# Maxima, squares and x in another order around the late joins of a fused attention and MoE kernel

## The reference

```python
for t in range(S):                       # attention: S = 768, 4 batches, 8 heads, D = 48
    S_re, S_im = (ar * S_re - ai * S_im + kv), (ar * S_im + ai * S_re)   # a normed to |a| <= 0.999
    y[:, :, t] = einsum('bhd,bhde->bhe', q[:, :, t], S_re)
x = y as (3072 tokens, 384)
h = maximum(maximum(x @ w1, x @ w2), x @ w3)    # 384 -> 768
x2 = h @ w_out                                  # 768 -> 384
expert = argmax(softmax(norm(x2) @ norm(emb).T / tau))   # 8 experts
out = gate * (relu(x2 @ e1[expert]) @ e2[expert])        # 384 -> 1024 -> 384
```

## Time and profile before

| | |
|---|---|
| median of three runs | 951.6 us |
| profiled execution | 952.29 us |
| its span | 950.6 us |
| mean granted TensorE clock | 0.948 |
| TensorE matmul busy | 841.3 us, 89% |
| VectorE busy | 662.6 us, 70% |
| GpSimd busy | 509.0 us, 54% |
| ScalarE busy | 441.8 us, 46% |

### The profile page before, as it was taken

How to read it: one execution, slowest core, us unless ns; L and a number is a source line. 1 busy time by engine, 2 the same in 40 slices (tenths; PEclk the granted TensorE clock), 3 DMA queues, 4 the chain that set the end, 5 groups by cost and what they waited for, 6 DMA issues and landing times.

```text
span 950.6 us, 18638 instructions
## 1 busy us (share of the span) xinstructions
PE 841.3 (89%) x6641; PEld 775.1 (82%) x6642; DVE 662.6 (70%) x1066; ACT 441.8 (46%) x817; POOL 509.0 (54%) x886
## 2 busy tenths in 40 slices
PE   0548898879898999999999999976999999999995
PEld 0436787779787988988888998875999999998894
DVE  5968898789888999999978756337623353647831
ACT  5676755646555556666543434221412132436611
POOL 1294989699997989899986000001332232324222
PEclk9777999989999999999999999995999999999998
DMA  9401141352424243423221111134721015245411
GB/s 305 110 20 31 29 141 64 91 142 73 111 72 105 74 106 100 107 69 92 77 60 39 40 41 48 48 115 157 280 69 50 33 52 183 66 152 204 144 34 42
DMA packets 41874, 89.72 MB, mean 94 GB/s; under 512 B 6264, under 2 KB 23680, under 8 KB 40480
## 3 DMA queue, kind: packets, MB, share of 16 engines
q1 hardware_dynamic: 37632, 76.04, 26.3%
q0 software_dynamic: 4160, 12.60, 4.0%
HBM read 69.74 MB, written 17.69 MB: 92 GB/s over the span
## 4 chain that ended last, share of the span: by engine, by line
PE 59%; DVE 22%; ACT 7%; issue 7%; DMA 2%; SPq 2%; ACTq 0%; DVEq 0%; POOL 0%; POOLq 0%
PE mm L1686 7%; PE mm L1690 6%; PE mm L1687 6%; PE yu L1686 4%; PE yu L1690 4%; PE yu L1687 4%; PE sc L1743 2%; DVE l_im L1136 2%; DVE l_re L1135 2%; PE tr L1954 2%; DVE h_sb L1155 2%; PE tr L1955 2%; PE mm L1955 2%; PE yu L1784 2%; PE mm L1954 2%
## 5 line engine op out<-in xcount | busy, mean ns | idle before, releaser
L1686 PE MATMUL mm<-up_hi,x_hi 128*128 128x384 f32 x432 | 159.3, 369 | 26.7 <-DVE h_sb L1155 13.7
L1687 PE MATMUL mm<-up_lo,x_hi 128*128 128x384 f32 x432 | 149.9, 347 | 0.0
L2053 POOL TENSOR_TENSOR c_re<-ring 112x128 f32<-112x128 f32 x165 | 101.3, 614 | 81.8 <-DVE ring L1108 48.3
L2054 POOL TENSOR_TENSOR c_im<-ring 112x128 f32<-112x128 f32 x165 | 119.0, 721 | 0.0
L1686 PEld LDWEIGHTS mm<-up_hi,x_hi 128*128 128x128 f32 x432 | 83.3, 193 | 41.7 <-DVE h_sb L1155 16.1
L2133 POOL DMA_INDIRECT out_rows<-g_o,rows_out x30 | 36.0, 1200 | 146.5 <-DVE g_o L1538 139.0
L1690 PE MATMUL mm<-up_hi,x_lo 128*128 128x384 f32 x432 | 102.3, 346 | 0.0
L2057 POOL TENSOR_TENSOR ring<-c_re,c_im 112x64 f32<-112x64 f32 x165 | 96.8, 586 | 0.0
L2109 POOL DMA_INDIRECT g_in<-x_scratch,rows_in x34 | 38.4, 1130 | 103.1 <-DVE rows_in L1501 77.6
L2056 POOL TENSOR_TENSOR ring<-c_re,c_im 112x64 f32<-112x64 f32 x165 | 80.5, 488 | 12.9
L1155 DVE TENSOR_TENSOR h_sb<-mm,h_sb 128x384 f32<-128x384 f32 x96 | 52.9, 552 | 49.2 <-PE mm L1690 47.1
(11 more groups left out here) (263 smaller groups left out, 2254.8 us busy)
## 6 DMA issues: line engine op xcount, KB each, us to landing
raw<-in_moe_w SPq DMA_DIRECT2D x16, 1536.0 KB, 9.2
a_dn<-in_a_laid SPq DMA_DIRECT2D x18, 384.0 KB, 6.9
an_scratch<-a_dn SPq DMA_DIRECT2D x18, 384.0 KB, 2.3
ring<-an_scratch SPq DMA_DIRECT2D x18, 384.0 KB, 5.3
q_in<-in_q_laid SPq DMA_DIRECT2D x24, 224.0 KB, 3.0
k_in<-in_k_laid SPq DMA_DIRECT2D x24, 224.0 KB, 3.2
v_in<-in_v_laid SPq DMA_DIRECT2D x24, 192.0 KB, 3.3
x_scratch<-x_sb SPq DMA_DIRECT2D x24, 192.0 KB, 2.3
```

Of the source, the lines that this page charges most:

```text
L1686: nc.tensor.matmul(out, hi[:, x, :], w_hi(x), start=(x == 0), stop=False)
L1687: nc.tensor.matmul(out, hi[:, x, :], w_lo(x), start=False, stop=False)
L2053: nc.gpsimd.tensor_tensor(c_re[:, 0:count, :, :], cur, bc(prev[:, :, 0, :], 2, 2), ALU.mult).then_inc(chain_prod, 1)
L2054: nc.gpsimd.tensor_tensor(c_im[:, 0:count, :, :], cur, bc(prev[:, :, 1, :], 2, 2), ALU.mult).then_inc(chain_prod, 1)
```

## The change

Five edits, in one table and in the lists of three engines:

- Group 3's joins: (3, 0) moves into the middle of round 4, (3, 1) behind its decays, and round 5 keeps only (3, 2). In rounds 3 and 5 the early joins stand ahead of the mask and the rotation.
- In a round with a late join (n in joins_late) VectorE takes both last maxima right behind the decays, then a norm_inverse, x_lo of this chunk, and only then the late join. The next round (called joined) leaves these out and takes both h_lo first.
- In a joined round ScalarE runs h_hi of the second half and the norm_rest put off by the round before ahead of stage_z; elsewhere the order of these stays.
- The square of a second norm in a round (rounds 4 and later) stands behind z_square.
- In a round with a late join, and in the last, SP moves only three of the six pieces of x (b = 0), and ScalarE's queue moves the other three behind the second moe_copy.

joins_late has the keys 2, 4, 6 and 8 to 20 after the change as before it, so the joined rounds are 3, 5, 7 and 9 to 21.

```diff
--- before.py
+++ after.py
@@ -485,13 +485,22 @@
         joins_late = {}
         joins_late[2] = [(2, 0)]
         joins_early[3] = [(2, 1), (2, 2)]
-        joins_late[4] = [(3, 0)]
-        joins_early[5] = [(3, 1), (3, 2)]
+        joins_early[4] = [(3, 0)]
+        joins_late[4] = [(3, 1)]
+        joins_early[5] = [(3, 2)]
         for g in range(4, NG):
             joins_early[2 * g - 2] = [(g, 0), (g, 1)] if g < 6 else [(g, 1)]
             joins_late[2 * g - 2] = [(g, 2)]
             if g >= 6:
                 joins_late[2 * g - 3] = [(g, 0)]
+
+        def shared_move(n):
+
+            return n in joins_late or n == NC - 1
+
+        def x_part(b, x):
+
+            return x_raw[HALF * b + D:HALF * (b + 1), x, :], y_end[HALF * b + x * GAP:HALF * b + (x + 1) * GAP, :]
 
         def router_bank(r):
             return mm if r % 2 == 0 else tr
@@ -568,9 +577,9 @@
 
             def move_x(n):
                 sp.wait_ge(y_copied, 2 * (n + 1))
-                for x in range(KX):
-                    for b in range(2):
-                        sp.dma_start(x_raw[HALF * b + D:HALF * (b + 1), x, :], y_end[HALF * b + x * GAP:HALF * b + (x + 1) * GAP, :]).then_inc(x_moved, 16)
+                for b in (0,) if shared_move(n) else range(2):
+                    for x in range(KX):
+                        sp.dma_start(*x_part(b, x)).then_inc(x_moved, 16)
 
             def load_up(x):
                 sp.dma_start(flat(up_raw[:, x, :, :]), w_up[x, :, :]).then_inc(up_loaded[x], 16)
@@ -850,18 +859,25 @@
                 norms = norms_in(n) if now else ()
                 later = norms_in(n + 1) if now else ()
                 late_z = n in (1, 3, 5)
+                joined = n - 1 in joins_late
                 if prev:
                     moe_x_hi(n - 1)
                 if prev2:
                     moe_h_hi(n - 2, 0)
-                for m in norms[1:]:
-                    norm_square(m, norm_of(m))
+                if n == 1:
+                    norm_square(7, norm_of(7))
+                if joined:
+                    moe_h_hi(n - 2, 1)
+                    for m in norms_in(n - 1):
+                        norm_rest(m, norm_of(m))
                 if more and not late_z:
                     stage_z(n + 1)
-                if prev2:
+                if prev2 and not joined:
                     moe_h_hi(n - 2, 1)
                 if more and not late_z:
                     z_square(n + 1)
+                for m in norms[1:] if n > 1 else ():
+                    norm_square(m, norm_of(m))
                 if n == 0:
                     norm_rsqrt(4, norm_of(4))
                 if prev:
@@ -899,7 +915,11 @@
                     low_copy(range(16, LOWS - KF))
                 if prev:
                     moe_copy(n - 1, 1)
-                for m in norms:
+                if now and shared_move(n):
+                    act.wait_ge(y_copied, 2 * (n + 1))
+                    for x in range(KX):
+                        act.dma_start(*x_part(1, x)).then_inc(x_moved, 16)
+                for m in norms if n not in joins_late else ():
                     norm_rest(m, norm_of(m))
 
             def steps(b):
@@ -1278,28 +1298,34 @@
                 norms = norms_in(n) if now else ()
                 ending = norms_in(n - 1) if 1 <= n <= NC else ()
                 late = joins_late.get(n, ())
-                if prev2:
+                joined = n - 1 in joins_late
+                if prev2 and not joined:
                     moe_max(n - 2, 1, 2)
                 if n == NC:
                     dve.wait_ge(low_step, 5)
                     nc.vector.tensor_copy(low[0:1, 0:1], sc[0:1, 0, 0:1]).then_inc(low_known, 1)
-                if prev:
+                if prev and not joined:
                     moe_x_lo(n - 1)
                 if prev2:
                     moe_h_lo(n - 2, 0)
+                if joined:
+                    moe_h_lo(n - 2, 1)
                 for m in ending:
                     norm_apply(m, norm_of(m))
                 for m in norms[:1]:
                     norm_m2(m, norm_of(m))
-                if prev2:
+                if prev2 and not joined:
                     moe_h_lo(n - 2, 1)
+                if n in (3, 5):
+                    for g, number in joins_early[n]:
+                        join(g, number)
                 if now:
                     mask(n)
                 if now and n >= 2:
                     rotation(n)
                 for m in norms[1:] if n >= 2 else ():
                     norm_m2(m, norm_of(m))
-                for g, number in joins_early.get(n, ()):
+                for g, number in joins_early.get(n, ()) if n not in (3, 5) else ():
                     join(g, number)
                 if n == 1:
                     rotation(n)
@@ -1326,14 +1352,21 @@
                 if more:
                     q_decay(n + 1)
                     k_decay(n + 1)
-                for g, number in late:
-                    join(g, number)
-                for m in norms:
+                if late:
+                    moe_max(n - 1, 1, 1)
+                    moe_max(n - 1, 1, 2)
+                for m in norms[:1]:
+                    norm_inverse(m, norm_of(m))
+                if late:
+                    moe_x_lo(n)
+                    for g, number in late:
+                        join(g, number)
+                for m in norms[1:]:
                     norm_inverse(m, norm_of(m))
                 if n == 0:
                     for m in (4, 5):
                         norm_apply(m, norm_of(m))
-                if prev:
+                if prev and not late:
                     moe_max(n - 1, 1, 1)
                 if n == NC - 2:
                     dve.wait_ge(fin_ready, NG)
```

## The result

The changed kernel takes 973.9 us (median of four runs, 972.97 to 975.32) against 951.9 (four runs, 950.55 to 953.77): a ratio of 1.023, 95% interval 1.021 to 1.026. It is slower, and the forecast was 976. The profiled execution took 973.05 us, 20.8 more than the one of before; its span is 970.9 us, 20.3 more.

The account below looks back on a forecast made before the run. TensorE, busy 89% of the span, was taken as the bound. Terms +16.8, +11.2, -2.0, +0.4, +2.5, +3.2 and -7.5 sum to +24.6 on 952.29, or 976.9; median forecast 976 us, range 968 to 984.

Parts of the forecast that it names:

- The term that counts: ScalarE, joined rounds: stage_z and norm rest behind h_hi delay its last down-product read 2.4 us in chunks 7, 9 to 16.
- That is covered, and I cost it at nothing: VectorE's later join: the last h_lo still ends before TensorE needs it; cost 0, or 0.5 us a chunk if uncovered.
- The slow clock: TensorE: each new wait of about 2.8 us is followed by slow clock costing 1.6 us; 11.2 in chunks 10 to 16.
- Rival A: The new mid-chunk waits don't drop the clock, so 1.6 us goes in each of ten chunks: 960 us; chance 0.12.
- Chunks 18 to 21, +3.2: ScalarE's last read of the down product: these chunks lose 0.8 us each, at full clock.
- Chunks 7 and 9, +0.4: New read wait and slow clock, 2.4 + 1.6, replace the old wait for the maxima and slow clock, 2.2 + 1.6.
- The early stretch, -7.5: Chunks 3 to 6 gain 7.5 us (2 to 12), limited by GpSimd's chain of group 4 gating chunk 6's join.
- Chunks 3 and 5 ... lose only the 0.6 us of the rest: ScalarE in chunks 3 and 5: they stage later anyway, losing only the 0.6 us norm rest, beside similar slack.
- x by two queues, 0: Three x transfers moved to ScalarE's queue cost 0; q, k, v loads start 1.8 us sooner; bounds under 0.5 us a chunk.
- B: ScalarE's late stage is absorbed, leaving only gains: 934 us; chance 0.06. The L769 wait row at 430.01 speaks against it.
- C: VectorE becomes the bound: 985 us, chance 0.05. Against it: ScalarE's wait stretches the chunk 4 us, giving VectorE room.
- D: The early gain comes whole, 12 us: 971 us, inside the forecast's own range and counted in its 0.73.

Follow-up runs that it names:

- ScalarE's order alone: Kernel before, with only the change's ScalarE order (second h_hi and put-off norm rest ahead of stage_z in joined rounds): 979.7 us.
- the stage put back: Changed kernel with stage_z again ahead of the second h_hi in joined rounds, norm rest still put off: 970.8 us.
- the two runs with the reads ahead there: New order in chunks 3 and 5 alone, down-product reads ahead of z_square and norm_mag in both, or in 5 only: 943.7 and 943.1 us.
- the three runs with the reads ahead in chunks 3 to 9 or everywhere: Down-product reads ahead: new order in chunks 3, 5, 7, 9 only, 943.4 us; all joined rounds, 944.4; the latter with last x by SP, 939.6.
- the runs with the reads ahead: Changed kernel, down-product reads and h_sb, kp copies ahead of z_square and norm_mag in all joined rounds: 944.4 us; with last x by SP 939.6.
- the last x by SP: Changed kernel with the last chunk's x moved by SP alone, as before the change: 971.8 us.
- all x by SP: Changed kernel with x moved by SP alone in every chunk, as before the change: 972.3 us.
- the run with chunks 3 and 5 and the reads ahead: New order in chunks 3 and 5 alone, with the down-product reads ahead of z_square and norm_mag in both: 943.7 us.
- the run with chunks 3 and 5 alone: Changed kernel with its new ScalarE and VectorE order in chunks 3 and 5 alone, two queues in chunks 2 and 4 alone: 944.4 us.
- the run with chunks 3 to 9: Changed order in chunks 3, 5, 7 and 9 alone, with the down-product reads ahead of z_square and norm_mag in these: 943.4 us.

## Why the prediction was right, and where it was not

**The term that counts, 2.4 us at the last read: right in size, half right in cause.** The waits of 2.8 us came in chunks 7 and 9 to 16, 1.75 in chunk 17 and 1.20 in 18 to 21, as forecast to 0.1 us. The 16.8 us of chunks 10 to 16 were 17.0. ScalarE's order alone makes them, as its run shows. But the step just ahead of it, "That is covered, and I cost it at nothing", on the join that comes later on VectorE, failed. I followed the join to h_lo alone. Behind h_lo stand the apply and norm_m2, and ScalarE's log waits for these ahead of z_all. With the stage put back that lateness, together with the norm rest still put off, came out at 1.65 to 2.2 us at the read in chunks 10 to 16, and at 1.0 to 1.4 us at h_hi in the odd ones. In the changed kernel ScalarE is later still, so VectorE's lateness cost nothing more, and the sum was right although a price in it was wrong. For the run with ScalarE's order put back the same working gave 942 us, and it takes 971.

**The slow clock, 1.6 us each: the price was right, the number was too high.** A chunk with a drop takes 1.5 us more than one without (25.51 against 24.02). Of the nine chunks with a wait of 2.8 us, the drop came in six: 7, 9, 10, 12, 15, 16. Chunk 17, with 1.75 us, had none. So chunks 10 to 16 lost some 5.8 us by the clock and not 11.2 (17.0 + 5.8, less 2.0 of old waits, make the 20.8 measured), and chunk 17 lost 0.8 and not 2.5. Rival A, that the clock holds, was true of some chunks.

**Chunks 18 to 21, +3.2:** measured +3.3. **Chunks 7 and 9, +0.4:** +1.4, since chunk 7 lost 2.7 us by the clock.

**The early stretch, -7.5: measured -6.9, but the limit was another one.** The prediction let GpSimd's chain of group 4 set it. The chain ended at 217.65 us, where GpSimd's rows turn to the next group:

```profile
176.66 0.46 POOL L2086 TENSOR_TENSOR c_re<-ring 112x128 f32<-112x128 f32 x1 [4.63 <-DMA ring<-an_scratch]
...
217.82 0.46 POOL L2086 TENSOR_TENSOR c_re<-ring 112x128 f32<-112x128 f32 x1 [0.17 <-POOL ring L2090]
```

VectorE came to the join 1.8 us later, without a wait:

```profile
219.47 0.68 DVE L1155 TENSOR_TENSOR l_re<-ring 112x512 f32<-112x512 f32 x1
```

The limit was chunk 5, where the prediction had seen "a new wait" only as its lower end: 4.42 us, because norm_mag waits for a norm_m2 behind a join and two applies. The step that failed is "Chunks 3 and 5 ... lose only the 0.6 us of the rest": the waits for that read were 2.00 and 4.42 us. When they are taken away VectorE itself holds chunk 5, as the two runs with the reads ahead there show. With more gained ahead of it, the gate is reached: VectorE's join of group 4 waited 0.2 to 0.5 us for GpSimd in the three runs with the reads ahead in chunks 3 to 9 or everywhere, and the join of group 6 1.85 to 5.80 us.

**x by two queues, 0: wrong in the last chunk.** +2.3 us of wait and 0.6 of slow clock more than before: the stretch took 34.90 us against 31.97. I had counted the loads that go ahead of ScalarE's pieces as q, k and v. In the last chunk they are the expert weights.

**The sum.** 19.5 us at chunk 23, and 2.9 in it, make 22.4; the rest of the span gave back 2.0, so 20.4 by the unrounded spans. In that rest the long waits are the same to 0.1 us (7.0, 3.1 and 2.6 us in the routing). All 2.0 us lie behind the routing, in the expert stage, where TensorE's waits sum to 7.1 us in both executions and the mean granted clock was 0.959 against 0.956. So I take them as spread of the clock; why it was higher was not shown. That forecast and median lie only 2 us apart is in part luck. The clock term was some 7 us too high (5.4 in chunks 10 to 16, 1.7 in chunk 17) and the 2.0 us given back were not foreseen. Against that stood 2.9 us that were missing in the last chunk, 1.0 in chunks 7 and 9, and 0.6 in the early stretch. That leaves some 4 us against the profiled execution, and the median lies 0.8 above that one.

**The rivals.** B (faster, the cover holds) failed as its contrary row said. C failed for the reason given, and the runs with the reads ahead show it as soon as ScalarE lets go: chunks 14 and 16 at 22.4 us. D, 12 us early, failed on chunk 5.

## What to carry to other kernels

When an engine's list is changed, follow its last late result through the other engine's list back to the reader that holds TensorE, and price each way as if the other were not there: two changes can each cost the whole amount, and then undoing one shows nothing. An instruction that holds a PSUM bank for TensorE belongs in front of anything that can wait for a third engine; moving three such reads, and two copies with them, turned a loss of 2.3% into a gain of 0.7%. Before a transfer is split over two queues, look at what the first queue issues next. And when a third engine works without a pause over several chunks, as GpSimd does here from 177 to 301 us, gains ahead of its next result count only up to that result.

## What the runs showed of the hardware

**The same wait drops the clock in one execution and not in the next.** With waits of 2.77 to 2.88 us for L778 in chunks 7 and 9 to 16, the granted clock fell below 1.00 in six of the nine chunks of the changed kernel, in two with the last x by SP, and in six with all x by SP. Chunks 15 and 13 of the run with the last x by SP, with 2.81 and 2.80 us:

```profile
426.08:450.13 24.05, 21.24 (x199) 19.41 (x198) 18.64 (x30) 13.10 (x26) 14.62 (x30) 1.00 0.35 89
376.51:402.06 25.55, 22.75 (x199) 20.72 (x198) 18.43 (x30) 13.12 (x26) 16.47 (x33) 0.93 0.42 105
```

The spread of one kernel's runs goes with the clock: with the last x by SP the run of 963.96 us had a mean clock of 0.954, the five of 971 to 974.6 us 0.940 to 0.947. A forecast should count such drops as a share and not as certain. Shorter waits are no safe side. In the run with ScalarE's order alone, two waits of 1.1 to 1.4 us in one chunk, 2.5 in sum, were followed by no drop in chunks 10 to 16. But a single wait of 1.49 us in chunk 13 was followed by one in the run with chunks 3 and 5 and the reads ahead, and by none in the run with chunks 3 and 5 alone. The two windows of chunk 13:

```profile
368.81:393.51 24.70, 22.84 (x199) 20.91 (x198) 21.59 (x35) 12.93 (x26) 22.07 (x41) 0.93 0.38 102
```

```profile
367.11:390.25 23.14, 21.28 (x200) 19.40 (x199) 21.31 (x35) 12.99 (x26) 20.98 (x38) 1.00 0.44 109
```

**GpSimd's steps are faster while VectorE stands still.** In the run with chunks 3 to 9, VectorE waits from 295.4 to 301.2 us, and the steps of the chain follow each other every 1.6 us:

```profile
296.38 0.46 POOL L2098 TENSOR_TENSOR c_re<-ring 112x128 f32<-112x128 f32 x1
...
298.03 0.45 POOL L2098 TENSOR_TENSOR c_re<-ring 112x128 f32<-112x128 f32 x1
...
299.65 0.45 POOL L2098 TENSOR_TENSOR c_re<-ring 112x128 f32<-112x128 f32 x1
```

The twelve steps of the same chain ahead of them, from 260.90 to 293.82 us, took 2.7 us each; VectorE was busy for 32.3 of those 32.9 us. In the changed kernel the 15 steps of group 4's chain took 2.5 us each (41.0 us from 176.66 to 217.65, less 3.4 of GpSimd's turn between them). The Trainium skill, in the rule on the shared port pair that the prediction draws on (SBUF — State Buffer), has VectorE instructions with two SBUF inputs and GpSimd instructions that read SBUF exclude each other. The trace agrees with it over three whole steps. No run here has a whole chain with VectorE idle: group 6's chain as a whole took 40.3 us in this run and 40.4 in the run with chunks 3 and 5 alone, where VectorE's first join of that group did not wait.
